# Two feed-forward layers behind windowed attention: seven products instead of eight in layer two, and another order of some of the work

## The reference

```python
scores = scale * np.matmul(q, k.transpose(0, 1, 3, 2))        # B=2, H=8, S=768, D=64
keep = is_sink | in_window                                    # 4 sinks, window of 128
a = softmax(where(keep, scores, -1e9));  x = a @ v            # x: 1536 x 512
h = x @ w_in;  g = np.maximum(0.01 * h, h);  y = g @ w_out    # layer one, d_ff 2048
h = y @ w_in2; g = h / (1 + np.exp(-h));  out = g @ w_out2    # layer two
```

## Time and profile before

| | us |
|---|---|
| median of 3 runs | 667.64 (667.15 to 668.63) |
| the profiled execution | 668.03 |
| its span, first to last instruction | 666.1 |
| TensorE busy | 638.8 |
| ScalarE busy | 299.9 |
| VectorE busy | 278.7 |
| GpSimd busy | 120.0 |

### The profile page before, as it was taken

One profiled execution on the slowest core, in us unless ns is written; L12 is line 12 of the kernel. 1 busy time (PEld: TensorE's weight loads), 2 busy tenths in 40 slices (PEclk: granted clock), 3 DMA queues, 4 the chain that ended last, 5 costly groups with the idle time before them and its releaser, 6 DMA issues.

```text
span 666.1 us, 9036 instructions
## 1 busy us (share of the span) xinstructions
PE 638.8 (96%) x3091; PEld 526.7 (79%) x3091; DVE 278.7 (42%) x646; ACT 299.9 (45%) x676; POOL 120.0 (18%) x165
## 2 busy tenths in 40 slices
PE   8886999999989999999999999999999999999997
PEld 4675787777868888887888888888888888888886
DVE  3897456555535655543222234333322222212222
ACT  4787556555545565543333344333323333223332
POOL 5786324232314333310000000000000000000000
PEclk8999999999989999999999999999999999999999
DMA  6565233433322123111011123223211212201201
GB/s 148 147 189 161 64 112 96 132 107 112 95 81 64 49 64 112 64 33 31 1 63 64 64 68 110 98 101 99 95 64 31 64 63 64 96 0 64 63 1 63
DMA packets 16941, 53.27 MB, mean 80 GB/s; under 512 B 2561, under 2 KB 2561, under 8 KB 16897
## 3 DMA queue, kind: packets, MB, share of 16 engines
q1 hardware_dynamic: 16512, 52.63, 25.7%
q10 hardware_dynamic: 384, 0.07, 0.1%
HBM read 49.55 MB, written 3.15 MB: 79 GB/s over the span
## 4 chain that ended last, share of the span: by engine, by line
PE 77%; issue 9%; DVE 5%; ACT 4%; POOL 3%; DMA 2%; SPq 0%; POOLq 0%; ACTq 0%; DVEq 0%
PE h_ps L805 37%; PE y_ps L831 33%; PE o_ps L771 2%; DMA qk_raw<-qk 2%; PE s_ps L726 1%; ACT prob L416 1%; PE t_ps L739 1%; DVE win L597 1%; DVE wout L603 1%; DVE att L591 1%; ACT wout L459 1%; POOL k_hl L336 1%; DVE g L608 1%; ACT q_st L427 1%; POOL x L315 1%
## 5 line engine op out<-in xcount | busy, mean ns | idle before, releaser
L805 PE MATMUL h_ps<-x,win 128*128 128x512 f32 x1152 | 284.4, 394 | 9.4 <-DVE win L597 5.2
L805 PEld LDWEIGHTS h_ps<-x,win 128*128 128x128 f32 x1152 | 214.0, 189 | 54.2 <-DVE win L597 6.8
L466 ACT ACTIVATE g_f<-h_ps 128x512 f32<-128x512 f32 x96 | 57.4, 598 | 269.8 <-PE h_ps L805 269.6
L831 PE MATMUL y_ps<-g,wout 128*128 128x512 f32 x576 | 146.5, 395 | 1.2 <-PE o_ps L771 1.2
L831 PE MATMUL y_ps<-wout,g 128*128 128x512 f32 x576 | 138.2, 390 | 0.0
L603 DVE TENSOR_TENSOR wout<-w_raw,wout 128x512 fp32r<-128x512 f32 x64 | 46.7, 729 | 192.0 <-ACT wout L459 192.0
L831 PEld LDWEIGHTS y_ps<-wout,g 128*128 128x128 f32 x576 | 108.2, 188 | 22.4
L831 PEld LDWEIGHTS y_ps<-g,wout 128*128 128x128 f32 x576 | 104.0, 188 | 20.6 <-issue 1.9
L608 DVE TENSOR_TENSOR g<-g_f,g 128x512 fp32r<-128x512 f32 x96 | 66.1, 689 | 99.4 <-ACT g L468 99.4
L416 ACT ACTIVATE prob<-sm,neg_max 128x260 f32<-128x260 f32 (+1 forms) x96 | 47.0, 490 | 52.7 <-DVE neg_max L546 52.6
L468 ACT ACTIVATE g<-h_ps 128x512 fp32r<-128x512 f32 x96 | 57.0, 593 | 0.0
(11 more groups left out here) (76 smaller groups left out, 407.4 us busy)
## 6 DMA issues: line engine op xcount, KB each, us to landing
w_raw<-w SPq DMA_DIRECT2D x64, 512.0 KB, 3.3
qk_raw<-qk SPq DMA_DIRECT2D x48, 260.0 KB, 4.4
v_raw<-vt SPq DMA_DIRECT2D x12, 256.0 KB, 3.7
y<-qk_raw SPq DMA_DIRECT2D x12, 256.0 KB, 2.3
vs_raw<-vsink ACTq DMA_DIRECT2D x8, 8.0 KB, 4.3
```

Of the source, the lines that this page charges most:

```text
L466: nc.scalar.activation(g_f32[:, F % 2, :], h_ps[:, :], func, alpha=slope)
L805: ins = mm(h_ps[:, :], win[:, split_slot[split_of[F]], wp, c * P:(c + 1) * P], x[:, xp, c, tokens(F)], start=(c == 0 and wp == HI and xp = ...
L831: ins = mm(y_ps[d][:, :], a[:, d * P:(d + 1) * P], r, start=(first and wp == HI and gp == HI), stop=(last and wp == LO))
```

## The change

Layer two's hidden product is done for a pair of slices at a time by Strassen's scheme. The two slices, the two halves of the input features and the two halves of the block's tokens make 2 x 2 blocks, and seven products take the place of eight. Each product is 2 input groups x 3 passes = 6 matmuls of 256 columns. The sums of weight blocks that the scheme needs (`w_sums`, four GpSimd operations for a pair: one of 512 elements, three of 256) and those of the tokens (`x_sums`, five of 512 for a block) are made on GpSimd, split by ScalarE and VectorE into `w7` (two copies by turns) and `xs`, and stand in memory that the attention and x leave free. The outputs are put together so: products for the off-diagonal blocks accumulate in one bank by turns (`h_ps`, `s_ps`), the shared product in `t_ps`; VectorE forms `d_sum`, `e_sum` and, for the diagonal blocks, `c_sum`. TensorE's queue runs this in three phases (18, 12 and 12 matmuls), with half of the pair's projection between them. In x's place layer one now leaves a plain float32 y (`y_f32`).

Layer two's weights are loaded for each pair and block, 48 slices instead of 32, and none stays. In layer one `KEPT` is 6 and 36 slices are split instead of 32.

The second part changes order: the two halves of the first k are subtracted apart, with the first two `mask_max` between them; sink columns are gathered once per half tile (a probability ring of 8, not 6); the first two slices are loaded and split earlier; and at the two block changes that lie in the attention (`turns`) the projection comes ahead of the next block's hidden product.

```diff
-    KEPT = 8
+    KEPT = 6
...
         if s < 2:
-            at, at_out = 3 * s - 5, 3 * s - 3
+            at, at_out = 5 * s - 14, 5 * s - 12
...
-    first_loads = (9, 11, 13, 15)
+    first_loads = (1, 6, 10, 14)
...
+        def turns(F):
+            return 0 <= F < LAST - FS and F % FT == FT - 1
...
+                    q = (j - RING - N_ONE) // 2
+                    sp.wait_ge(w_sum, 4 * (q + 1))
+                    sp.wait_ge(w7_ready, 3 * q + 1)
                 wait(sp, wout_ready, j - RING + 1)
...
+            def sum_weights(q):
...
+                nc.gpsimd.tensor_tensor(to[:, A11_A12:A11_A12 + 2, :], raw[:, :, 0, :], raw[:, :, 1, :],
+                                        ALU.add).then_inc(w_sum, 1)
+                nc.gpsimd.tensor_tensor(to[:, A21_A11, :], two[:, 1, :], one[:, 0, :],
+                                        ALU.subtract).then_inc(w_sum, 1)
...
+            def sum_x(b, i):
...
+                nc.gpsimd.tensor_tensor(x_sums[:, i % 2, :, :], y_part(b, k0, n0), y_part(b, k1, n1), op).then_inc(xs_sum, 1)
...
+            for q in range(NPF):
+                if q + 2 < NPF:
+                    sum_weights(q + 2)
+                b, i = divmod(q, FP)
+                if b + 1 < NB and i < 7:
+                    sum_x(b + 1, i)
...
+                if turns(F):
+                    evacuate(F, 1)
+                    take_hidden(F + 1)
...
+            def take_diagonal(q):
+                act.wait_ge(c_ready, q + 1)
...
+                nc.scalar.activation(g_f32[:, 1, :], src, ACT.Silu)
+                nc.scalar.activation(g2[:, q % 2, 0, 2:4, :].rearrange("p i n -> p (i n)"), src,
+                                     ACT.Silu).then_inc(b_taken, 1)
...
+            def low_xs(b, i):
+                dve.wait_ge(xs_high, 7 * b + i + 1)
+                src = x_sums[:, i % 2, :, :] if i < 5 else y_part(b, i - 5, i - 5)
+                nc.vector.tensor_tensor(x_part(b, i, 1), src, x_part(b, i, 0).bitcast(F32), ALU.subtract).then_inc(xs_ready, 1)
+            def shared(q):
+                dve.wait_ge(m_done, 3 * q + 1)
+                xy = xy_bank(q)
+                nc.vector.tensor_reduce(d_sum[:, :], xy[:, :].rearrange("p (i n) -> p n i", i=2), mybir.AxisListType.X,
+                                        ALU.add).then_inc(d_ready, 1)
+                dve.wait_ge(d_ready, q + 1)
+                nc.vector.tensor_tensor(e_sum[:, :], z_ps[:, 0:2 * P], d_sum[:, :], ALU.subtract).then_inc(e_ready, 1)
+            def sum_diagonal(q):
+                dve.wait_ge(m_done, 3 * q + 3)
...
+                nc.vector.tensor_tensor(c_sum[:, :, :], xy_bank(q)[:, :].rearrange("p (i n) -> p i n", i=2),
+                                        e_sum[:, :].unsqueeze(1).to_broadcast([P, 2, 2 * P]),
+                                        ALU.add).then_inc(c_ready, 1)
...
+                if a == 0:
+                    low_first_k(1)
...
+            def product(q, w_i, x_i, to, start, stop=False):
+                for c in range(2):
+                    for wp, xp in PASSES:
+                        ins = mm(to, w_part(q, w_i, 1, wp)[:, 0, c * P:(c + 1) * P], x_part(q // FP, x_i, xp)[:, c, :],
...
+            def strassen(q, phase):
...
+                if phase == 0:
+                    pe.wait_ge(w7_ready, 3 * (q + 1))
...
+                    product(q, A11_A22, B11_B22, z_ps[:, 0:2 * P], True, True)
+                    product(q, A11_A12, B22, c12, True)
+                    ins = product(q, A22_A21, B11, c21, False)
+                elif phase == 1:
+                    pe.wait_ge(e_ready, q + 1)
+                    product(q, A11, B12_B22, c12, False)
+                    ins = product(q, A22, B21_B11, c21, False)
+                else:
+                    pe.wait_ge(a_taken, q + 1)
+                    product(q, A21_A11, B11_B12, c12, False, True)
+                    ins = product(q, A12_A22, B21_B22, c21, False, True)
...
-                hidden(F + 1, 0)
+                if not turns(F):
+                    hidden(F + 1, 0)
...
+            strassen(0, 0)
+            project(NSTEP - 1, 0)
+            strassen(0, 1)
+            project(NSTEP - 1, 1)
+            strassen(0, 2)
+            for q in range(NPF):
+                if q + 1 < NPF:
+                    strassen(q + 1, 0)
+                project_pair(q, False)
+                if q + 1 < NPF:
+                    strassen(q + 1, 1)
+                project_pair(q, True)
+                if q + 1 < NPF:
+                    strassen(q + 1, 2)
```

More of the change, by code:

```diff
@@ L1 @@
 from contextlib import ExitStack
+from math import prod
 import concourse.bass as bass
@@ L60, in sink_window_attention_two_ffn @@
             first_step.append(F)
-        j = resident[layer, f]
+        j = resident[f]
         split_of.append(j)
         if F % FT < FT - KEPT or b == NB - 1:
-            del resident[layer, f]
+            del resident[f]
             free.append((split_slot[j], F))
+    N_ONE = len(split_w)
+    for q in range(NPF):
+        for i in range(2):
+            slot, left = free.pop(0)
+            split_w.append((1, 2 * (q % FP) + i))
+            split_slot.append(slot)
+            slot_left.append(left)
+        free += [(split_slot[N_ONE + 2 * q + i], NSTEP + q) for i in range(2)]
     NSPLIT = len(split_w)
+    assert N_ONE % RING == 0
     FS = PAIRS * TB + 3
-    first_loads = (9, 11, 13, 15)
+    first_loads = (1, 6, 10, 14)
     LAST = NPAIR + 4
@@ L284, in _ @@
                 load_ws(F)
-                i, f = divmod(F - N_L0, FT)
-                if i > 0 and f == 1:
-                    store(i - 1)
+            for q in range(2, NPF):
+                for i in range(2):
+                    load_w(N_ONE + 2 * q + i)
+                if q - 4 >= FP and (q - 4) % FP == 1:
+                    store((q - 4) // FP - 1)
             store(NB - 1)
@@ L656, in _, with low_first_k @@
             nc.vector.memset(prob_sink[:, :, :, :, :], 0.0).then_inc(zeroed, 1)
-            for half in range(2):
+            def low_first_k(half):
                 dve.wait_ge(k_high, half + 1)
@@ L688, in _ @@
                     low_wout(s)
-                if not head:
+                if not head and not turns(F):
                     low_g(F + 1)
@@ L700, in _ @@
                     low_g(F + 1)
+                else:
+                    shared(0)
+                    low_pair_g(0, 0)
                 for s in win_in.get(F, ()):
                     low_win(s)
+                if X_TICK <= F < X_TICK + 7:
+                    low_xs(0, F - X_TICK)
+                if F >= TAIL and F % 2 == 0:
+                    low_w7((F - TAIL) // 2)
+                if F >= TAIL:
+                    low_wout(N_ONE + F - TAIL)
                 evacuate(F, 0)
             evacuate(NSTEP - 1, 1)
+            for q in range(NPF):
+                store_half(q - 1, 1)
+                sum_diagonal(q)
+                low_pair_g(q, 1)
+                if q + 1 < NPF:
+                    shared(q + 1)
+                if q + 2 < NPF:
+                    low_w7(q + 2)
+                b, i = divmod(q, FP)
+                if b + 1 < NB and i < 7:
+                    low_xs(b + 1, i)
+                if q + 1 < NPF:
+                    low_pair_g(q + 1, 0)
+                if q + 2 < NPF:
+                    for i in range(2):
+                        low_wout(N_ONE + 2 * (q + 2) + i)
+                store_half(q, 0)
+            store_half(NPF - 1, 1)
         @block.tensor
@@ L792, in hidden @@
             def hidden(F, half):
-                layer, b, f = steps[F]
+                b, f = steps[F]
                 if half == 0:
@@ L822, in project @@
                 for d in (2 * half, 2 * half + 1):
-                    if first and blk:
-                        if blk <= NB:
-                            pe.wait_ge(y_ready, 4 * (blk - 1) + d + 1)
+                    if first and b:
+                        pe.wait_ge((y_act, y_dve)[d % 2], 2 * (b - 1) + d // 2 + 1)
+                    for wp, gp in PASSES:
+                        ins = mm(y_ps[d][:, :], wout[:, split_slot[split_of[F]], wp, d * P:(d + 1) * P],
+                                 g[:, gp, F % 2, :],
+                                 start=(first and wp == HI and gp == HI), stop=(last and wp == LO))
@@ new lines, in project_pair @@
+            def project_pair(q, diagonal):
+                b, i = divmod(q, FP)
+                pe.wait_ge(wout_ready, N_ONE + 2 * q + 2)
+                pe.wait_ge(gp_ready, 2 * q + 1 + diagonal)
+                first, last = i == 0 and not diagonal, i == FP - 1 and diagonal
+                for d in range(TB):
+                    s, at = ((0, 3), (0, 3), (1, 2), (1, 2))[d] if diagonal else ((1, 1), (1, 1), (0, 0), (0, 0))[d]
+                    if first:
+                        if b == 0:
+                            pe.wait_ge((y_act, y_dve)[d % 2], 2 * (NB - 1) + d // 2 + 1)
```

307 lines of the change are left out of this document (239 added, 68 removed).

## The result

The changed kernel takes 672.46 us (median of 9 runs, 669.79 to 674.80) where the kernel before, run beside it, takes 667.86 (9 runs, 666.42 to 669.95). The ratio is 1.0068, with a 95% interval of 1.0050 to 1.0087: slower by 4.6 us. The prediction was 661.7 us, with a range of 653.5 to 671. The profiled execution of the changed kernel took 674.15 us (span 672.4), 1.7 above its median. What follows compares it with the profiled execution of before (668.03, span 666.1), so that it has 6.1 us to explain where the medians have 4.6.

What follows compares the result with a forecast made beforehand. TensorE was taken to bound layer two, busy 50.00 of 50 us. Layer two -3.2, block changes -2.2 and start -0.5 gave -5.9 on the profiled 668.03: 662.1, or 661.7 at the median, range 653.5 to 671.

Steps and rivals of the forecast that it cites:

- layer two: Strassen rounds on TensorE: -11.6 us, plus 7.0 for 14 rounds, 1.2 for output copies, 0.2 for the last round: -3.2.
- the block changes: Layer one's changes inside the attention: -2.6 us at the first, +0.4 at the change to block 2, together -2.2.
- the start: Kernel start with k halves apart and earlier weight loads and splits: -0.5 us taken, between +2 and -2.
- The entry into layer two "has slack": Passage from layer one to two: table load and splits lie beside layer one's last steps; a bare table load costs 1.28.
- The x sum falls beside c and its idle: Layer two rounds that prepare x: GpSimd's token sum runs beside VectorE's c and its idle, adding nothing to VectorE's round.
- 14 rounds lose 0.5, the output copies 1.2: Layer two: VectorE's 10.9 us rounds with an xs lose 7.0 in all; output copies at two block ends lose 0.6 each.
- TensorE's pace: Layer two's round on TensorE: 42 narrow matmuls at 0.118 us and 24 wide at 0.2267, 10.40 instead of 10.88.
- The lock between VectorE and GpSimd: Two-source SBUF operations exclude each other, PSUM ones do not; a GpSimd sum holds 1.17 us at 512 elements, 0.60 at 256.
- both new waits: First block change: scores(69) waits 0.6 us for mask_max(68), hidden(17) 1.1 on ScalarE; the new wait at block 2 is 1.3.
- Rival B: Layer two: each GpSimd sum costs VectorE its whole hold, so VectorE's round becomes the clock; +16.2 there, 681.1 us; chance 0.15.

Runs made afterwards that it cites:

- entry move: Changed kernel with d_sum and e_sum of the first pair ahead of the second pair's w7 and wout subtractions at layer two's entry: 670.52 us, ratio 1.0042.
- the seven: The seven profiles of kernels with the new start, changed kernel included: first hidden product begins at 68.53 to 69.60 us.
- mended kernels: Changed kernel with VectorE's d and e earlier at the entry and wout subtractions behind c, five variants of start and turns: medians 659.70 to 661.34 us.
- the old start: Changed kernel with first weight loads, split ticks and both first k subtractions as in the kernel before: 672.16 us, ratio 1.0066.
- wout moved: Changed kernel with VectorE's two wout subtractions of a round moved behind the next round's c: 663.21 us, ratio 0.9940.
- thin token sums: Changed kernel with GpSimd's token sums covering 8 columns instead of 256 from the second block on: 666.33 us, ratio 0.9981.

## Why the prediction was wrong

The sum had layer two at -3.2, the block changes at -2.2 and the start at -0.5. The profiled executions have +4.9, then -0.5 (-1.9 and +0.2 at the changes, +1.1 and +0.1 behind them), and +1.9 (+2.9, of which 1.0 is made up by hidden(15)). By its steps:

- **The entry into layer two "has slack": in the profile this step failed most, by 4.0 us** (11.72 against the 7.7 of its matmuls at the paces predicted). I looked at ScalarE's cover, and the table load was hidden as expected (1.28 us at 400.53), but I didn't follow VectorE's order: four low parts blocked by GpSimd stood ahead of d and e, on which phase 1 waits. 2.1 us were idle and the rest was mostly the half clock behind it. The entry move takes the whole of it out of the profile (7.96), and 1.9 us out of the medians.
- **"The x sum falls beside c and its idle": refuted.** It comes right behind the four weight sums. Without it the kernel is 6.1 us faster, so in the medians this step, booked at nothing, failed most. With it, the slowest rounds take 11.9 us, not the 10.9 predicted.
- **14 rounds lose 0.5, the output copies 1.2: right in its sum by luck.** Counting 10.51 as free, the 22 rounds lost 240.67 - 231.2 = 9.5 us, against 8.2. Fifteen of them took over 10.55, six of these 11.3 or more, and eight 10.8. Without the x sums they lost 234.72 - 231.2 = 3.5: what was booked at 8.2 cost 3.5, and the x sum, booked at nothing, 6.0.
- **TensorE's pace: 10.51 a round, not 10.40.** The narrow matmuls were 0.119 (0.118 taken), worth 0.04, and the wide ones, which I had left at 0.2267, were 0.2296, worth 0.07. Over 24 rounds it is 2.6 us. What slows the wide ones beside narrow ones was not tested. By the Trainium skill (TensorE: Matmul & The Clock Gate, Back-to-back issue gap) the narrow ones would be 262 cycles, 0.109 us at 2.4 GHz; no stretch here reached that.
- These terms, 4.0 + 1.3 + 2.6, and a rest of 0.2, are the 8.1 us between -3.2 and +4.9.
- **The lock between VectorE and GpSimd: right** in its kind and its prices. The weight sums meet w7, xs, g and wout; PSUM operations keep their time; d takes 0.68 (0.69 taken), e 0.42 (0.40). TensorE's waits stand on e alone. The Trainium skill (SBUF — State Buffer, "SBUF: two separate sides") has it that the loser is blocked for the whole of the other's instruction; the round of VectorE shown above agrees, with VectorE's 512-wide operations ending 0.55 us behind each sum.
- **The block changes: right in the places looked at, wrong behind them.** -1.9 and +0.2 against -2.6 and +0.4, with both new waits as described (0.62, and 1.02 to 1.27 on ScalarE). But 1.6 us of the first (19.66 against 18.09) was a fall of the clock that not every execution has, and the stretch behind it, booked at nothing, takes 1.1 us more; what in it waits was not traced. In the kernel before the turns are worth 0.1 us, in the changed kernel both together about 0.8. The second one by itself costs 0.4 in the traces (13.69 and 81.73 against 13.43 and 81.60); the medians have 0.8 (660.49 against 659.70), from two groups.
- **The start: wrong in sign.** Instead of -0.5 it is +2.9 at the first hidden product, outside its bounds of -2 to +2, and +1.9 by hidden(15); that execution has the latest start of the seven. The early loads and splits cost about 1.6 us in the medians of the mended kernels and only 0.3 where VectorE's rounds were late anyway.

Rival B named the right mechanism: VectorE's round as the clock, decided from a mean round of 11.0 us on. The mean round was 10.94, just under that, and the 22 rounds together took 1.3 us more than before; the entry and the start, which B left as they were in the forecast, did the rest. I gave B 0.15, because I placed the x sum in an idle without following GpSimd's queue: it comes behind four sums that end when VectorE is at wout.

Left open: why the changed kernel's runs spread from 669.8 to 674.8 us while those of the four mended ones that have a turn lie within 0.3 to 0.9. Only one execution of each was profiled. A half clock that comes and goes with the waits of 2 us doesn't order them: the changed kernel has 672.46 at a mean clock of 0.995 and 670.91 at 0.992, the kernel with the entry move 671.36 at 0.997 and 667.15 at 0.992. Both still have the crowded rounds, and the four mended ones don't; more isn't shown. The 2.9 us of the start weren't traced to single waits.

## What to carry to other kernels

Work given to GpSimd is not free because GpSimd is idle: each of its SBUF operations that meets two-source SBUF work of VectorE adds most of its time to VectorE's queue (VectorE's 512-wide subtraction went from 0.69 to 1.23 us beside a sum of 0.73, and to 1.78 beside one of 1.29), so place by queue order, not by busy share, which VectorE operations they meet, and put those with a PSUM source or a wait there. Where a loop takes over from another one, follow each engine's order at the seam by itself: one late value cost 4.0 us there in the profile and 1.9 in the medians, where 22 rounds of the loop lost 9.5. And take a gain that rests on a clock dip in one execution only once a second one shows it, and measure such a gain to the end of the stage: what the turn gained at the change it gave back behind it.

## What the hardware did that I had not expected

- With both queues full, VectorE and GpSimd took turns operation by operation: five sums in a row (1.78, 1.45, 1.19, 1.19, 1.74 us, alone 1.29 and 0.73) against five subtractions of 1.22 to 2.05 us (0.69 when 512 wide, 0.95 when 768 wide, without full sums beside them). Neither ran two in a row until the other's queue was empty.
- An idle of 2.09 us on TensorE behind a stretch of full work in the entry was followed by 3.4 us at half clock in the changed kernel, and by a fall of the clock too with the old start (0.73 from 403 to 407 us) and with wout moved (0.68 from 407 to 412), but not with thin token sums (1.00), though the wait there was the same. The 2.64 us wait for x was followed by half clock in two of the three profiles that have it.
- The reduce over pairs in PSUM took 0.68 us for 512 inputs, as long as a two-input operation of that size.
- Wide matmuls of a projection come 0.2296 us apart on average when groups of narrow ones lie between them, and 0.2267 when all are wide; the surplus is in the first five.
